# Twelve additions of the decay preparation issued by GpSimd in place of VectorE

## The reference

```python
mag = np.sqrt(a_re * a_re + a_im * a_im)
scale = np.minimum(mag, 0.999) / (mag + 1e-06)
a_re_n, a_im_n = (a_re * scale, a_im * scale)
for t in range(S):
    ar, ai = (a_re_n[:, :, t, :, None], a_im_n[:, :, t, :, None])
    new_re = ar * S_re - ai * S_im
    new_im = ar * S_im + ai * S_re
    kv = np.einsum('bhd,bhe->bhde', k[:, :, t], v[:, :, t])
    S_re, S_im = (new_re + kv, new_im)
    y[:, :, t] = np.einsum('bhd,bhde->bhe', q[:, :, t], S_re)
# x = y as 3072 x 384 tokens
h = x @ w_in
solu = h * softmax(h)
ln = (solu - mu) / np.sqrt(var + 1e-06) * g_ln
x = ln @ w_out
# gates, top 2 of 8 experts, out += weight * (relu(x @ w1[e]) @ w2[e])
```

## Time and profile before

| | |
|---|---|
| median of three runs | 1130.34 us (1128.93 to 1134.17) |
| the profiled execution's own time | 1130.34 us |
| its span, first to last instruction | 1128.6 us |
| mean granted TensorE clock | 0.950 |
| busy: PE, PEld, DVE, ACT, POOL | 992.8, 923.3, 842.6, 639.6, 402.6 us |

### The profile page before, as it was taken

How to read it: one execution, slowest core, us unless ns; L and a number is a source line. 1 busy time by engine, 2 the same in 40 slices (tenths; PEclk the granted TensorE clock), 3 DMA queues, 4 the chain that set the end, 5 groups by cost and what they waited for, 6 DMA issues and landing times.

```text
span 1128.6 us, 20986 instructions
## 1 busy us (share of the span) xinstructions
PE 992.8 (88%) x7460; PEld 923.3 (82%) x7460; DVE 842.6 (75%) x1572; ACT 639.6 (57%) x1081; POOL 402.6 (36%) x389
## 2 busy tenths in 40 slices
PE   0446899999989989999956999999999999999896
PEld 0245798888878978979846999999999999999895
DVE  5799999899899888645554777676776786777582
ACT  6754666866866735645443565565565565555461
POOL 4012132243343343344533344334343423443422
PEclk9867899999999989999976999999999999999898
DMA  9521131231231111221407867767677667767620
GB/s 237 195 90 36 35 102 31 70 92 44 57 92 58 44 36 56 48 60 30 134 15 266 284 210 251 277 243 245 240 279 255 240 233 282 252 240 255 220 80 20
DMA packets 84823, 167.43 MB, mean 148 GB/s; under 512 B 17417, under 2 KB 56544, under 8 KB 84720
## 3 DMA queue, kind: packets, MB, share of 16 engines
q1 hardware_dynamic: 72336, 137.60, 37.7%
q0 software_dynamic: 12288, 28.39, 6.9%
q10 hardware_dynamic: 96, 0.10, 0.0%
HBM read 146.46 MB, written 20.74 MB: 148 GB/s over the span
## 4 chain that ended last, share of the span: by engine, by line
PE 43%; DMA 10%; issue 6%; DVE 4%; ACT 2%; POOL 1%; POOLq 0%; DVEq 0%; ACTq 0%; SPq 0%
PE bank L1563 13%; PE bank L1764 10%; DMA prev<-out,mine 6%; PE bank L1624 5%; PE bank L1672 4%; PE bank L1554 3%; DMA out<-yo,mine 3%; PE bank L1792 2%; PE bank L1646 2%; DVE yo L1502 2%; PE bank L1684 2%; DVE w1l L1241 1%; ACT z L991 1%; POOL out L740 1%; ACT w1h L825 0%
## 5 line engine op out<-in xcount | busy, mean ns | idle before, releaser
L1032 ACT ACTIVATE hh<-bank 128x256 fp32r<-128x256 f32 x200 | 76.8, 384 | 219.3 <-PE bank L1563 219.3
L1563 PE MATMUL bank<-sxh,w1h 128*128 128x256 f32 x600 | 172.1, 287 | 2.1 <-DVE sxl L1490 2.1
L1563 PE MATMUL bank<-sxh,w1l 128*128 128x256 f32 x600 | 170.0, 283 | 0.0
L1563 PE MATMUL bank<-sxl,w1h 128*128 128x256 f32 x600 | 169.8, 283 | 0.0
L1509 DVE SCALAR_TENSOR_TENSOR hl<-bank,hh 128x256 fp32r<-128x256 f32 x200 | 84.6, 423 | 91.8 <-ACT hh L1032 91.8
L1764 PE MATMUL bank<-w2h,hh 128*128 128x384 f32 x400 | 136.3, 341 | 8.0 <-DVE hl L1509 7.9
L740 POOL DMA_INDIRECT out<-yo,mine x56 | 67.5, 1206 | 205.7 <-DVE yo L1502 196.4
L1764 PE MATMUL bank<-w2l,hh 128*128 128x384 f32 x400 | 135.0, 337 | 0.0
L1764 PE MATMUL bank<-w2h,hl 128*128 128x384 f32 x400 | 134.8, 337 | 0.0
L1247 DVE TENSOR_TENSOR w2l<-raw,w2h 128x768 fp32r<-128x768 f32 x124 | 117.5, 961 | 21.6 <-ACT w2h L830 21.0
L1241 DVE TENSOR_TENSOR w1l<-raw,w1h 128x1024 fp32r<-128x1024 f32 x93 | 112.4, 1221 | 20.1 <-ACT w1h L825 19.8
(11 more groups left out here) (237 smaller groups left out, 2541.7 us busy)
## 6 DMA issues: line engine op xcount, KB each, us to landing
raw<-in_w SPq DMA_DIRECT2D x62, 1536.0 KB, 8.6
ar<-in_a_re SPq DMA_DIRECT2D x6, 768.0 KB, 4.8
turn<-in_a_im SPq DMA_DIRECT2D x6, 768.0 KB, 6.6
qk<-in_q SPq DMA_DIRECT2D x48, 96.0 KB, 2.4
qk<-in_k SPq DMA_DIRECT2D x48, 96.0 KB, 2.5
out<-wide SPq DMA_DIRECT2D x9, 512.0 KB, 12.3
vt<-in_v SPq DMA_DIRECT2D x24, 192.0 KB, 2.6
xs<-x SPq DMA_DIRECT2D x24, 192.0 KB, 2.7
```

The source lines that it names most:

```text
L1032: nc.scalar.activation(hh[:, f % NH, :], bank[:, f % 2, 0:CAP], ACT.Relu).then_inc(hh_done, 1)
L1563: ins = MM(dst, stationary[a_](cc), moving[b_](cc), start=(n_ == 0), stop=(n_ == len(terms) - 1))
```

## The change

The four adds of each of the chunks c = 1, 2 and 3 are issued by POOL. The functions `m2` and `zsum` and their semaphores are as before; `m2_later` and `zsum_later` are gone from DVE.

```diff
@@ POOL, body(c, b, n) @@
-                if b == 3 and c == 0:
+                if b == 1 and 0 < c < C - 2:
+                    m2(2 * c + 4)
+                if b == 3 and c + 2 < C:
                     zsum(2 * c + 5)
...
                 if c == 0 and b == 1:
                     m2(2 * c + 4)
-                if b == 1 and c == 0:
+                if b == 1 and c + 2 < C:
                     zsum(2 * c + 4)
-                if b == 2 and c == 0:
+                if b == 2 and c + 2 < C:
                     m2(2 * c + 5)
@@ DVE @@
-            def m2_later(q):
-                dve.wait_ge(sq_done, 2 * (q + 1))
-                V.tensor_tensor(mag(q, 0), mag(q, 0), mag(q, 1), ALU.add).then_inc(m2_done, 1)
...
-                if b == 1 and 0 < c < C - 2:
-                    m2_later(2 * c + 4)
                 if b == 3 and prep:
                     state_decays(c + 1)
-                if b == 3 and 0 < c < C - 2:
-                    zsum_later(2 * c + 5)
...
                 if has(n):
                     q_products(n)
-                if b == 1 and 0 < c < C - 2:
-                    zsum_later(2 * c + 4)
-                if b == 2 and 0 < c < C - 2:
-                    m2_later(2 * c + 5)
```

More of the change, by code:

```diff
@@ L1167, in state_decays @@
                 V.tensor_tensor(md[:, 0:NG, :, 2], v[0][:, 1], v[1][:, 1], ALU.subtract).then_inc(m_step, 1)
-            def m2_later(q):
-                dve.wait_ge(sq_done, 2 * (q + 1))
-                V.tensor_tensor(mag(q, 0), mag(q, 0), mag(q, 1), ALU.add).then_inc(m2_done, 1)
-            def zsum_later(q):
-                dve.wait_ge(ln_done, 4 * (q + 1))
-                V.tensor_tensor(mag(q, 0), mag(q, 0), mag(q, 1), ALU.add).then_inc(z_sum, 1)
             def norm(q):
```

## The result

| | before | after |
|---|---|---|
| median of the runs beside each other | 1132.26 us (1128.93 to 1134.61, 4 runs) | 1144.64 us (1143.67 to 1147.95, 4 runs) |
| ratio of the runs, 95% interval | | 1.0131 [1.0106, 1.0154] |
| the profiled execution's own time, its span | 1130.34, 1128.6 us | 1144.36, 1142.6 us |
| mean granted TensorE clock | 0.950 | 0.945 |

A forecast was written before the change was run, and what follows sets the result against it. PE sets the pace in some bodies, DVE in two of four. Losses of 1.9, 1.6 and 0.95 us in chunks 1 to 3, together 4.45 us, on 1130.34 us give 1134.8 us; range 1128.0 to 1140.0.

The forecast's parts named there:

- B: Second sum of the first half, end of b = 1: DVE 0.45 us later, all on the path, in each chunk.
- C: First sum of the second half, end of b = 2: starts under xl, holds qp; 0.35, 0.35, 0 us by chunk.
- D: Second sum of the second half, b = 3: POOL's masking and state operations move back, norm held; 0.8, 0.8, 0.3 us.
- A: First sum of the first half, b = 1: holds one running-product row 1.5 us; costs 0.3, 0, 0.2 us by chunk.
- Stretched rows in b = 1: Sign: under POOL's adds, DVE rows of 192 elements take 1.5 to 1.9 us in place of 0.36.
- stretched qp in b = 2: Sign: qp, after xl, is held to the end of POOL's add, done at about 197.2 in place of 196.08.
- PE's wait for kp of over 1 us in body 7: Sign: PE's waits before kp in bodies 7 and 11 reach 1 us and more; body 7 had 0.32.
- Rival 3: All twelve meetings cost 0.63 us, D 0.8 us per chunk, and the clock falls: 1142.1 us; chance 0.20.
- Rival 2: DVE's loss is covered by PE's pace, or loss and gain cancel: 1130.3 us, give or take 2; chance 0.15.
- Rival 1: Holding is rare in the new places, six adds' 0.87 us is kept, 5.2 us: 1125.1 us; chance 0.10.

The follow-up runs named there:

- B alone: Against the kernel before, only the second sum of the first half (end of b = 1, chunks 1 to 3) moved to POOL; 1.0051 [1.0017, 1.0086].
- D alone: Against the kernel before, only the second sum of the second half (b = 3, chunks 1 to 3) moved to POOL; 1133.67 us, a single execution.
- A alone: Against the kernel before, only the first sum of the first half (b = 1) moved to POOL; 1135.84 us once, 1.0022 [0.9999, 1.0045] in repeated runs.
- C alone: Against the kernel before, only the first sum of the second half (end of b = 2, chunks 1 to 3) moved to POOL; 1.0004 [0.9978, 1.0031].
- all narrow: All twelve adds on POOL as in the change, each adding only 16 of 768 columns (results incomplete); 1.0007 [0.9984, 1.003] to the kernel before.
- the kernel whose masking waits: The changed kernel, with POOL's masking of each b = 2 made to wait for the three norm rows; 1.0072 [1.0043, 1.01] to the kernel before.
- both waits: The changed kernel, with b = 2's masking waiting for norm and the second half's first sum waiting for qp; 1.0045 [1.0024, 1.0065] to the kernel before.

## Why the prediction was wrong

**Right.** That DVE's rows with two SBUF operands are held by POOL's adds, and for how long; that PSUM rows aren't; that DVE's busy time would not fall; that the time goes in the first stage. (The prediction said this of all rows whose operands are in SBUF. That is too wide: a reciprocal of one SBUF operand kept its 0.15 us under POOL, as shown at the end.) Right as well is B's own price to DVE: 0.45 us, and the gap went from 1.17 to 0.72 in all three chunks with B alone. C's own, 0.35 us, is in order too: alone, qp grows by 1.04 to 1.13 us and an add of 0.87 us is gone, so 0.17 to 0.26 us a time are left. D's 0.8 us is what D alone shows in two chunks of three. From body 17 on the kernel mostly only moved, give or take 1.5 us beside the 2.25 us of bodies 20 to 21.

**The step that failed** is the sum itself: each add was priced at the alignment of the trace of before, and the prices were added. Its words on A, "DVE itself is 0.6 us later (1.5 - 0.87), which its own waits at the end of the body cover", and on B, that "all 0.45 us are on the path", end the account with DVE's lateness. They don't ask which of POOL's existing rows DVE meets after a shift of that size. Its margin there was under 0.15 us (nothing held at 1.16, a row held at 1.02). So B's 0.45 us cost 0.9 us more at norm, with A's on top 1.54, and then, as a second consequence, C started 1.7 us behind kp and not 2.6, and cost 1.6 us at xl rather than 0.35 at qp. In chunk 1, kp lies 10.33 us behind norm's start (before 9.46) and xl 4.71 us behind kp (before 3.09): 0.87 + 1.62 = 2.5 us of the 3.5 us that the stretch grew. Over the three chunks these two terms make 7.4 of the 9.6 us, where the prediction had nothing at norm in b = 2 and 0.35, 0.35 and 0 us for C. Another 1.8 us is the lateness with which DVE comes to norm, 1.35 us of it B's own three times 0.45, which was priced. That leaves 0.4 us in sum behind xl, +0.50, -0.09 and -0.01 us by chunk. The clock fell in these stretches from 1.00, 1.00 and 0.92 to 0.87, 0.93 and 0.93. By an estimate (one less the clock, times the length) that is 5.1 us of PE's work more than before, out of 6.4 us over the whole span (0.950 of 1128.6 us, 0.945 of 1142.6). But DVE sets the pace in them, and what is left over is 0.4 us, so the fall is a consequence here and hardly a cost. The 4.4 of the 14.0 us outside the three stretches stay in part unexplained.

**Sizes.** From the masking of b = 1 to that of the next b = 0, in chunks 1, 2 and 3, the prediction had 1.9, 1.6 and 0.95 us; the profiles show 4.2, 2.2 and 2.9 us. The b = 0 to b = 1 stretches, for which it had nothing, show 2.0 us in sum, but with one of them shorter (25.56 to 23.89), so their share isn't settled. A's lateness, put at 0.6 us, is 0 to 0.22 us in the gaps of A alone. D's 0.8 us was right for chunk 2 (norm held by 0.74 us). In chunks 1 and 3 ACT's copy waited 1.26 and 1.23 us for PE, norm was not held, and it started 4.11 us behind the copy's end in place of 3.88: 0.2 us. The prediction allowed for that wait in chunk 3 alone, and at its length before, 0.37 us.

**Its signs.** Stretched rows in b = 1 showed. The stretched qp in b = 2 did not: the carry rows ahead of xl were stretched instead, and that difference was readable at once as the fault. PE's wait for kp of over 1 us in body 7 did not come either, since PE, late from body 6, reached kp at 217.81, after kp's 216.40 plus its length.

**The rivals.** Rival 3 (more, with a clock drop: 1142.1 us, chance 0.20) is nearest, by 2.5 us, and the clock did fall as it says, from 0.950 to 0.945 in the mean. Its mechanism, all twelve meetings at the full 0.63 us and D at 0.8 in each chunk, is not what happened: C alone would then have shown 1.9 us in the three stretches, and they grew by 0.45 in sum. That its time is near is luck. Rival 2 (hidden) holds for C alone. Rival 1 (gain) is refuted even in its best case: with next to nothing to hold, all narrow is 1.0007 [0.9984, 1.003]. Its 5.2 us took DVE's time between B and L1140 for the kernel's; the three stretches of that profile were shorter (4.1 us), and the whole was not.

The Trainium skill, "GPSIMD Engine Reference", section 1 (Specifications), has contention where a VectorE instruction has two SBUF inputs, and the held norm rows (1.44 and 1.20 us) agree with it. Which side waits, and that a masking with a single input holds DVE as an add does, the traces above show.

## What to carry to other kernels

Where two engines exclude each other, don't price a moved operation by what it holds where it lands: take the lateness that it gives the other engine, shift that engine's rows by it in the trace, and look for every existing meeting further on whose order turns. Write down the margin of each such meeting first, here 0.15 us at the masking and 0.4 us at xl; a shift larger than a margin costs the whole hold, not the shift. Test a sum of parts by pairs, since what costs nothing alone (C, 1.0004) cost half of the loss in company. It goes the other way too: D's 0.8 us shrank to 0.2 where another delay had already moved the masking.

## What the runs showed of the hardware

The exclusion has two sides, and in these rows the one that starts first keeps its time. In chunk 1 after, the masking at 182.42 was 0.06 us ahead of a norm row: it took 1.09 us and the row 1.44. In chunk 3 a norm row at 357.56 was 0.01 us ahead of the masking at 357.57: the row took 0.55 us and the masking 1.49. A DVE row with a single SBUF input is not held. In the kernel before, body 6, the reciprocal runs inside a decay operation of POOL, and the product row behind it is held (DVE, POOL):

```profile
185.95 0.15 DVE L1384 RECIPROCAL esum<-esum 128x1 f32<-128x1 f32 x1
186.02 1.13 DVE L1134 TENSOR_TENSOR turn<-cum 128x384 f32<-128x384 f32 x1
...
185.57 1.16 POOL L641 TENSOR_TENSOR st<-state,md 128x384 f32<-128x384 f32 x1
```

POOL's successive operations don't shut DVE out as a block: between the masking and the decay of the state one norm row got through (182.48, ended 183.92, the masking ended 183.51). And TensorE's clock stood at 0.87 and 0.93 in stretches where PE had waited 1.8 to 3.9 us in front of its gate product, and at 1.00 in the first stretch of the kernel whose masking waits, where that wait was 0.89 us; with both waits it was 0.94 us at a mean of 0.92. PE's wait for xl is no better sign: it was 3.04 us in that stretch at 1.00. These are means over a stretch, and from one profile each; no rule of the clock comes out of them.
